# Expert slots of a gated mixture: tokens turned by VectorE's block transposes and an exchange through DRAM in place of TensorE's transposes

## The reference

```
# expert layer
for each token s of batch b:
    e = argmax(logits[b, s]), or the expert of the token before, by a local gate
    h = maximum(x[b, s] @ w1[e], 0)          # 512 -> 1024
    out[b, s] = p[e] * (h @ w2[e])           # 1024 -> 512
# last layer
h = maximum(x @ w_in, 0); conv over 3 neighbours; gate = sigmoid(conv)
out = (h * gate) @ w_out
```

## Time and profile before

| | |
|---|---|
| median of 3 runs | 746.84 us (746.83 to 748.22) |
| span of the profiled execution | 746.1 us |
| PE busy | 735.4 us |
| DVE busy | 432.8 us |
| ACT busy | 322.1 us |
| POOL busy | 329.1 us |

### The profile page before, as it was taken

How to read it: one execution, slowest core, us unless ns; L and a number is a source line. 1 busy time by engine, 2 the same in 40 slices (tenths; PEclk the granted TensorE clock), 3 DMA queues, 4 the chain that set the end, 5 groups by cost and what they waited for, 6 DMA issues and landing times.

```text
span 746.1 us, 15123 instructions
## 1 busy us (share of the span) xinstructions
PE 735.4 (99%) x4971; PEld 626.7 (84%) x4971; DVE 432.8 (58%) x1042; ACT 322.1 (43%) x635; POOL 329.1 (44%) x442
## 2 busy tenths in 40 slices
PE   8999999999989999999999999999999999999998
PEld 6788887887887888888888888888899889889986
DVE  5777878878776544444444545454399455636510
ACT  5777878878430112212121311100397345535620
POOL 7759788887325469444444854400521100000000
PEclk9999999999999999999999999999999999999999
DMA  7888879984064666333334543200421110000011
GB/s 161 206 211 224 230 204 217 239 223 124 17 200 142 232 193 249 144 127 142 127 141 127 171 160 119 89 29 29 139 62 33 43 36 15 29 29 14 29 43 56
DMA packets 99848, 93.39 MB, mean 125 GB/s; under 512 B 62124, under 2 KB 71620, under 8 KB 99780
## 3 DMA queue, kind: packets, MB, share of 16 engines
q1 hardware_dynamic: 79252, 46.51, 22.9%
q10 hardware_dynamic: 17056, 34.69, 13.6%
q0 software_dynamic: 3472, 11.28, 5.3%
HBM read 76.13 MB, written 16.33 MB: 124 GB/s over the span
## 4 chain that ended last, share of the span: by engine, by line
PE 70%; DVE 1%; DMA 0%; issue 0%; ACT 0%; POOLq 0%; DVEq 0%; ACTq 0%
PE row_bank L1306 19%; PE wide_bank L1289 18%; PE wide_bank L1551 14%; PE row_bank L1589 13%; PE wide_bank L1327 3%; PE bank L1255 1%; PE bank L1520 1%; DMA x_slots<-x_rows,token_of 0%; PE bank L1540 0%; PE wide_bank L28 0%; PE row_bank L1540 0%; PE bank L1017 0%; DVE y_sb L1411 0%; DVE xs_tr L1376 0%; DVE xs_tr L1374 0%
## 5 line engine op out<-in xcount | busy, mean ns | idle before, releaser
L912 POOL TENSOR_TENSOR ring<-raw_w,ring 128x2048 fp32r<-128x2048 f32 x28 | 128.6, 4614 | 87.7 <-ACT ring L902 87.7
L1289 PE MATMUL wide_bank<-ring,xs_tr 128*128 x600 | 143.3, 394 | 0.7 <-DVE xs_tr L1368 0.4
L1306 PE MATMUL row_bank<-ring,h_tr 128*128 x600 | 143.5, 394 | 0.0
L902 ACT ACTIVATE ring<-raw_w 128x2048 fp32r<-128x2048 f32 x30 | 55.8, 1908 | 200.3 <-DMA raw_w<-in_moe_w_dram 169.6
L1306 PEld LDWEIGHTS row_bank<-ring,h_tr 128*128 128x128 f32 x600 | 110.8, 188 | 22.7
L1289 PEld LDWEIGHTS wide_bank<-ring,xs_tr 128*128 128x128 f32 x600 | 110.7, 188 | 22.9 <-issue 1.1
L1551 PE MATMUL wide_bank<-x_tr,ring 128*128 128x288 f32 x768 | 107.7, 297 | 0.0
L1551 PEld LDWEIGHTS wide_bank<-x_tr,ring 128*128 128x128 f32 x768 | 103.2, 188 | 0.9
L1589 PE MATMUL row_bank<-ring,g_tr 128*128 128x512 f32 x432 | 100.1, 389 | 0.0
L1589 PEld LDWEIGHTS row_bank<-ring,g_tr 128*128 128x128 f32 x432 | 80.5, 188 | 16.1
L692 ACT ACTIVATE prob<-score,row_min 128x128 f32<-128x128 f32 (+2 forms) x144 | 83.4, 580 | 17.9 <-DVE row_min L555 14.6
(11 more groups left out here) (236 smaller groups left out, 1009.5 us busy)
## 6 DMA issues: line engine op xcount, KB each, us to landing
raw_w<-in_moe_w_dram ACTq DMA_DIRECT2D x12, 2048.0 KB, 8.8
ncum_row<-cum_rows SPq DMA_DIRECT2D x15, 512.0 KB, 5.6
y_sorted<-y_sb SPq DMA_DIRECT2D x26, 256.0 KB
raw_w<-in_moe_w_dram SPq DMA_DIRECT2D x12, 512.0 KB, 3.9
ncum_tail<-cum_rows SPq DMA_DIRECT2D x32, 144.0 KB, 4.4
out_dram<-out_sb ACTq DMA_DIRECT2D x18, 256.0 KB, 2.0
v_nat<-in_v_dram SPq DMA_DIRECT2D x32, 128.0 KB, 3.0
q_nat<-in_q_dram SPq DMA_DIRECT2D x30, 128.0 KB, 4.0
```

Source lines behind the costliest of these rows:

```text
L902: nc.scalar.activation(high, whole, ACT.Copy).then_inc(high_ready, 1)
L912: nc.gpsimd.tensor_tensor(low, whole, high.bitcast(F32), ALU.subtract).then_inc(low_ready, 1)
L1289: last = nc.tensor.matmul(h_bank[:, half, :], xs_tr[:, a, kb, :], ring[:, bass.ds(n, 1), b, at:at + FH].rearrange("p a c -> p (a c)"), sta ...
L1306: last = nc.tensor.matmul(y_bank[:, :], h_tr[:, a, kb, :], ring[:, bass.ds(n, 1), 2 + b, kb * D:(kb + 1) * D].rearrange("p a c -> p (a c)" ...
```

## The change

The tokens of slots 2 to 24 are no longer turned by TensorE.

- SP writes each gathered slot to the new DRAM tensor `x_turn` (256 KB) and reads it back with four DMAs, one for each 32 partitions: partition 32 g + r gets, from each of the four tokens r, r + 32, r + 64, r + 96, the 128 columns from 128 g on. These pieces are 512 bytes long. The read of a slot is issued after the write of the next one.
- DVE then transposes blocks of 32 x 32 within its groups of 32 partitions (`V.transpose` into `late`), with every fourth column in one block row. After that, the copy and the subtraction run as before, but from `late` in SBUF and not from PSUM (`move_x_blocks`).
- The turned tokens now have column 4 p + k in partition p, block k, in place of column 128 k + p. So w1 of every expert is loaded with whole rows, rows 4 p to 4 p + 3 in partition p; w_in stays as it was. TensorE turns slots 0 and 1 as before, but takes every fourth column.
- `turn_x` leaves the loop of TensorE. The loops of DVE and SP are written out.
- On SP the stores of y of slots 0, 1 and 2 stand behind parts of the exchange: `y_store(0)` behind the write of slot 9, `y_store(1)` behind that of 14, `y_store(2)` behind that of 19, all later ones behind the whole exchange.

```
-        with sp.Fori(0, SLOTS - 1) as s:
+
+        def x_write(s):
+            n, i = s % 2, (s - BY_PE) // 2
+            sp.wait_ge(slot_loaded[n], 16 * (s // 2 + 1))
+            above(sp, x_out[n], 16 * i)
+            sp.dma_start(x_turn[s], x_slots[:, s, :]).then_inc(x_out[n], 16)
+
+        def x_read(s):
+            n, i = s % 2, (s - BY_PE) // 2
+            sp.wait_ge(x_out[n], 16 * (i + 1))
+            above(sp, x_back[n], 16 * QUARTERS * i)
+            for g in range(QUARTERS):
+                sp.dma_start(x_slots[g * Q:(g + 1) * Q, s, :].rearrange("p (i c) -> p i c", i=QUARTERS),
+                             x_turn[s][:, g * P:(g + 1) * P].rearrange("(i r) c -> r i c", r=Q)).then_inc(x_back[n], 16)
+
+        def y_store(s):
             sp.wait_ge(y_ready, s + 1)
-            sp.dma_start(y_sorted[bass.ds(s * P, P), :], y_sb[:, :]).then_inc(y_stored, 16)
+            sp.dma_start(y_sorted[s * P:(s + 1) * P, :], y_sb[:, :]).then_inc(y_stored, 16)
+
+        def x_swap(begin, end):
+            for s in range(begin, end):
+                if s < SLOTS:
+                    x_write(s)
+                if BY_PE <= s - 1:
+                    x_read(s - 1)
+
+        x_swap(BY_PE, 10)
+        y_store(0)
+        x_swap(10, 15)
+        y_store(1)
+        x_swap(15, 20)
+        y_store(2)
+        x_swap(20, SLOTS + 1)
+        for s in range(3, SLOTS - 1):
+            y_store(s)
...
+    def every_fourth(s, kb):
+        return x_slots[:, s, :].rearrange("p (c k) -> p k c", k=KD)[:, kb, :]
...
         for s in range(1, SLOTS - 1):
             hidden(s, loaded=n if s == 1 else None)
-            turn_x(s + 1, (s + 1) % 2, (s + 1) // 2)
             output(s - 1)
             turn_h(s)
...
+        def move_x_blocks(s):
+            dve.wait_ge(x_back[s % 2], 16 * QUARTERS * ((s - BY_PE) // 2 + 1))
+            dve.wait_ge(xs_ready, s)
+            V.transpose(late[:, :].rearrange("p (k i r) -> p k i r", k=KD, i=QUARTERS),
+                        x_slots[:, s, :].rearrange("p (i c k) -> p k i c", i=QUARTERS, k=KD)).then_inc(x_blocks, 1)
+            dve.wait_ge(x_blocks, s - BY_PE + 1)
+            dve.wait_ge(h_done, 2 * s)
+            turned = late[:, :].rearrange("p (k c) -> p k c", k=KD)
             V.tensor_copy(xs_tr[:, 0, :, :], turned).then_inc(xs_high, 1)
             dve.wait_ge(xs_high, s + 1)
             V.tensor_tensor(xs_tr[:, 1, :, :], turned, xs_tr[:, 0, :, :].bitcast(F32), ALU.subtract).then_inc(xs_ready, 1)
...
-        with dve.Fori(1, SLOTS - 1) as s:
+        for s in range(1, SLOTS - 1):
             relu(s)
-            move_x(s + 1)
+            move_x_blocks(s + 1)
             move_y(s - 1)
             move_h(s)
```

More of the change, by code:

```diff
@@ L769, in attention, with mixture @@
     return sync_part, pool_part, tensor_part, vector_part, scalar_part, x_stored, X_STORES, logit_ready, x_ready
-def mixture(nc, ctx, sems, region, identity, attend, x_rows, y_sorted, w_gate, w_local, w1, w2, w_in, conv_w, w_out, out):
+def mixture(nc, ctx, sems, region, identity, attend, x_rows, y_sorted, w_gate, w_local, w1, w2, w_in, conv_w, w_out, out, x_turn):
     N, D = x_rows.shape
@@ L878, in mixture @@
                          "tokens_sorted"))
[L879 removed]
+    slot_ready, tails_apart = sem("slot_ready"), sem("tails_apart")
     conv_turned, conv_ready = sem("conv_turned"), sem("conv_ready")
@@ L957, in sync_between @@
             rows = (D, F)[w] // 4
+            source = matrix[quarter * rows:(quarter + 1) * rows, :].rearrange("(c p) f -> p c f", p=P) if w else \
+                matrix.rearrange("(p c) f -> p c f", c=KD)[:, quarter:quarter + 1, :]
             sp.dma_start(raw[n][w][:, quarter * (WE // 4):(quarter + 1) * (WE // 4)].rearrange("p (c f) -> p c f", f=width),
-                         matrix[quarter * rows:(quarter + 1) * rows, :].rearrange("(c p) f -> p c f", p=P)).then_inc(first_loaded[part], 16)
+                         source).then_inc(first_loaded[part], 16)
     def sync_route(sp):
@@ L1113, in vector_route @@
         slot_tokens(1)
-        V.tensor_copy(place_i[:, :], place[:, :]).then_inc(place_ready, 1)
+        V.tensor_copy(place_i[:, :], place[:, :])
         then(V.tensor_scalar(tiles_upto[:, 1:1 + E], tiles_upto[:, 1:1 + E], 1.0 / P, None, ALU.mult))
@@ L1181, in mixture @@
     HK = KF // 2
+    Q = 32
+    QUARTERS = P // Q
+    BY_PE = 2
+    x_out, x_back = [sem(f"x_out{n}") for n in range(2)], [sem(f"x_back{n}") for n in range(2)]
+    x_blocks = sem("x_blocks")
     FH = F // 2
@@ L1217, in next_weights @@
             act.wait_ge(h_done, 2 * slots)
-            load_weights(act, n, 0, first)
+            load_weights(act, n, 0, first, e is not E)
             high_parts(act, n, i, 0)
@@ L1254, in turn_x @@
             for kb in range(KD):
-                last = nc.tensor.transpose(x_bank[:, kb * P:(kb + 1) * P],
-                                           x_slots[:, s, kb * P:(kb + 1) * P], identity[:, :])
+                last = nc.tensor.transpose(x_bank[:, kb * P:(kb + 1) * P], every_fourth(s, kb), identity[:, :])
             last.then_inc(xs_turned, 1)
@@ L1263, in turn_first_x @@
                 at = kb % 2 * P
-                last = nc.tensor.transpose(bank[kb // 2][:, at:at + P], x_slots[:, 0, kb * P:(kb + 1) * P], identity[:, :])
+                last = nc.tensor.transpose(bank[kb // 2][:, at:at + P], every_fourth(0, kb), identity[:, :])
                 if kb == 1:
@@ L1760, in program @@
     y_sorted = dram("y_sorted", (slots * P, D))
+    x_turn = dram("x_turn", (slots, P, D))
     with ExitStack() as keep:
@@ L1770, in program @@
         att, mix = mixture(nc, always, keep, region, identity, attend, x_rows, y_sorted,
-                           w_gate, w_local, w1, w2, w_in, conv_w, w_out, out)
+                           w_gate, w_local, w1, w2, w_in, conv_w, w_out, out, x_turn)
         keep.callback(region.close)
```

12 lines of the change are left out of this document (8 added, 4 removed).

## The result

| | median of the runs, us | range | ratio to before (95%) |
|---|---|---|---|
| before | 746.84 | 746.68 to 748.22 (5 runs) | |
| after | 809.73 | 807.91 to 819.4 (5 runs) | 1.0863 (1.0813 to 1.0914) |

The kernel became 63 us slower; I had said 16 slower, with 780 as the upper end. The profiled execution of after is its longest run, 819.4 us, with a span of 817.7 against 746.1 before: 71.6 us to account for.

What follows compares the result with a forecast made beforehand. TensorE, busy for 99% of the span, was taken to bound the kernel. 746.1 - 10.0 (turnings) + 16.3 (late gathers) + 10.1 (DVE beside POOL) = 762.5 us of span, 763.2 us for the run; range 738 to 780.

Steps and rivals of the forecast that it cites:

- 23 x 0.436 = 10.0 us off the path: TensorE's chain: 23 turnings of slot tokens leave the loop, each worth 0.44 us, 10.0 us saved.
- So the last gather at 282: POOL's gathers, sharing the DMA engines with the exchange: the last comes 16 us later (ends 4 and 26), near 282.
- Stall 16.3 us, once: TensorE before hidden(5): waits once for the third expert's late w1 low parts, done at 292.6 but wanted at 276.3.
- behind the stall of the next paragraph it is hidden: y_store(3) behind the exchange on SP: alone a wait of 0 to 12 us, covered by the stall from late gathers.
- the exchange itself sets the pace: Rival, chance 0.12: gathers 26 us late or more, or 512-byte pieces costing double, y_store(3) 28 us late; 775, up to 785.
- 2.5 us each, 10.1 in all (ends 0 and 16): DVE's copy and subtraction wait for POOL's low-part pairs at four w1 loads (experts 4, 5, 6, w_in), delaying hidden.
- end before they cost TensorE anything: POOL's other pairs of low parts, laid beside the shorter rounds: no cost to TensorE.
- The trace's 1.52 us says it waits through both: An attention DVE pass over SBUF, median 0.17 us, took 1.52; so DVE's copy waits through both passes of POOL's pair.
- about 1.8 us each, 7 in all: The skill's port rule read strictly: the copy enters after POOL's first pass, only the subtraction waits for the second.
- an output and a turning cover 6.4 us: After relu(s), output (5.49) and turning of h (0.87) cover DVE's three new passes, 1.9 us, at no cost.
- That w1 is loaded in whole rows ...: nothing: The w1 weight loads: whole rows change which rows land where, not their bytes, so no cost.
- The clock: TensorE's granted clock, 1.00 through the stage before; a fall in the long stall would make the prediction too low.

Runs made afterwards that it cites:

- the version without waits: Against the changed kernel: transpose written to PSUM, exchange paced by y stores, low parts of the third expert's w1 and w2 made before the last gathers; 735.79 us, 0.985 of before.

## Why the prediction was wrong

The direction and both mechanisms were right, and 16 us were foretold where 63 came. Step by step:

- **"23 x 0.436 = 10.0 us off the path"**: right, a little small. Rounds are 0.50 shorter, because output too went from 5.49 to 5.44; the version without waits gains 11.05.
- **"So the last gather at 282", "Stall 16.3 us, once"**: right in its mechanism and its size, 284.07, and 17.15 us of stall once the stores were out of the way. In after it never showed: the low parts were done at 294.2, and TensorE, held up by the stores, came to hidden(5) at 293.7.
- **"behind the stall of the next paragraph it is hidden"**: the first step that failed. I had priced the fourth store, and the three that stand inside the exchange at nothing. They came first: the stores of slots 0 and 1 were issued 5.8 and 13.2 us after their y was there, because SP was at the exchange, and landed after 12.4 and 9.8 us, where the prediction took 2. I had taken that landing as if nothing ran beside it, though the same paragraphs put the DMA engines at a share of 0.9 and loads of w1 there. The exchange was through at 312.7 (282 to 302 was said), 3.8 us a slot and not 3. The waits of output are 13.6 us in after, and 27.4 where nothing else stood before them. The rival "the exchange itself sets the pace" came nearest, with 0.12: it had SP through at 317, but it too had the fourth store late and not the first two.
- **"2.5 us each, 10.1 in all (ends 0 and 16)"**: the step that failed most. The sharing was real, and its place was mostly elsewhere. The four pairs that were meant (experts 4, 5, 6 and w_in) cost 8.4 us, 2.1 each, where 10.1 was said; the fifth pair of first weights, expert 7's, cost 4.37 more. The pairs of second weights, which "end before they cost TensorE anything", cost 16.5: I had not laid the copy beside each of them row by row. And I never laid it beside the low parts that pile up behind the gathers, though the prediction itself had put them there: 19.5 us. With the slower matmuls behind these waits, moving the tile to PSUM is worth 38.3 us.
- **"The trace's 1.52 us says it waits through both"**: half right. Where it weighs the other reading, at "about 1.8 us each, 7 in all", its own terms give 2.0 each (2.5 less the copy's 0.5), and 2.1 was measured. In pairs the copy went in between (1.58 us) and the subtraction waited for the second pass. That is as the Trainium skill has it (SBUF — State Buffer, SBUF: two separate sides): the pair of ports goes to whichever instruction starts first, for that instruction. The trace agrees for the pairs. It does not for the row of six, where the copy stood through the rest of the first pass and five whole ones. The same section limits the lock to DVE's two-port modes and to two SBUF inputs; here too the trace agrees, since the transpose (one SBUF input, 1.07 to 1.13 us in all 23) and passes that read PSUM never waited.
- **"an output and a turning cover 6.4 us"**: right for the passes themselves. The transpose took 1.10 and not 0.69, within its ends, and cost nothing.
- **"That w1 is loaded in whole rows ...: nothing"**: wrong, 7.3 us. The first store landed 4.1 us sooner without them, but the waits of output did not shrink; the trace has the difference at the pairs, and how the rows bring it about is not shown.
- **The clock**, named only as what would make it too low: 15.5 us of slower matmuls. In after a stall of 3.5 us or more has such a term of 1.4 to 2.6 us for the next group alone. The nine groups behind the waits at pairs took 12.7 us more than nine of 5.7, beside 29.3 us of waits. It belongs in the sum beside every stall.

So the error is not one number. 10.1 us stood for a cost of some 38, and a wait held to be hidden was one of 13.6 us, 27.4 once the tile was in PSUM.

## What to carry to other kernels

Where a PSUM bank is free, try a DVE result that DVE reads again there when POOL works on SBUF at the same time: the place of one tile was worth 38 us here. Lay such a pass beside every group of the other engine, those that pile up behind a late step above all, and not only beside the pairs that look closest. Transfers that run ahead should be paced by what uses them up, one for each slot, and a single-buffered store must not stand behind them in a queue's program (here it stood there for 6 to 20 us); then look at the next smallest spare (here 1.5 us behind the gathers), because that is the wait which appears next.

## What the runs showed of the hardware that I had not expected

- An SBUF-to-SBUF copy of DVE that takes 0.43 us took 24.9, 26.5, 26.2 and 27.4 us beside the row of POOL's passes behind the gathers, with passes of 4.5 us as with passes of 1.25 us. Beside four passes in a row later in the slots it took 4.1 us. The block transpose of 512 columns, SBUF to SBUF, never took longer than 1.13 us beside them.
- A block transpose with a strided source can write PSUM, in 1.09 us at the median: the same as into SBUF.
- A 256 KB store, issued among the exchange's transfers on SP's queue, landed after 12.4 us beside a 2 MB load in rows of 16 KB on ACT's queue, and after 8.4 us beside the same load in rows of 4 KB. This is one execution of each; with rows of 16 KB two other kernels had 10.5 and 13.0 us at that place.
- Of TensorE's waits in the slots of all these kernels, those of 3.5 us and more were followed by a group of 24 products that took 7.1 to 8.6 us in place of 5.6 to 5.7, those under 1.2 us were not, and of those around 2 us some were and some were not (2.22 us: 7.32 once, 5.71 once). What decides there stays open.
